# Attention of tile 0 moved ahead of preparation 1, weight splits and raw buffers reordered, a first slot of its own

## The chip, the cores and the metric

The kernel runs on one core of one Trainium2 chip. The metric is the time of one execution on the device in microseconds. All arithmetic is float32; large products are done as three float32r products of high and low parts.

## The reference

Three stages follow one another. The first is a recurrence over 768 tokens for 4 x 8 heads of 48 channels; the second and third are dense layers over the 3072 tokens.

```python
scale = np.minimum(mag, 0.999) / (mag + 1e-06)      # mag = sqrt(a_re^2 + a_im^2)
for t in range(S):
    new_re = ar * S_re - ai * S_im                  # a times the state, complex
    new_im = ar * S_im + ai * S_re
    S_re, S_im = new_re + kv, new_im                # kv = outer(k_t, v_t)
    y[:, :, t] = q_t @ S_re
h = x @ w_in                                        # 384 -> 2048
x = (np.maximum(h, 0) + np.log1p(np.exp(-np.abs(h)))) @ w_out   # -> 384
out = (((x @ w1) * (x @ w2)) @ w3) @ w_out2         # 384 -> 1024 -> 384
```

## The kernel before

The 3072 tokens are cut into eight tiles of 384 tokens. For each tile there are three kinds of work. A *preparation* makes the running products of a (log and root on ScalarE, some 46 us of elementwise work on VectorE), from which q times p and k divided by p are made, stored and loaded back in another layout (stq, stk). The *attention* of a tile has six parts i (three chunks by two groups of heads): `scores` and transposes and `outputs` on TensorE, `mask_scores` and `new_state` on VectorE, `k_by_tokens` and `y_out` on ScalarE, then `store_y` by DMA into x1raw. The *dense layers* of a tile take eight steps j: `up(n, j)` projects x1 by w_in, `softplus` (three passes, ScalarE), `add_relu` (VectorE, L1192), `g_high` (ScalarE, L762), `g_low` (VectorE, L1199) and `down(n, j)` multiplies by w_out.

Engines run their instructions in the order in which they are written, and that order is written by hand. A slot n holds the dense layers of tile n, the attention of tile n + 1 (parts 0 to 5 at steps 0 to 5), the preparation of tile n + 2 and the head of that of tile n + 3. On TensorE a step is `up(n, j+1)`, `scores(n+1, j)`, `down(n, j)`, `outputs(n+1, j)`. The last output product of a slot, `down(n, 7)`, is done in the next slot.

Ahead of slot 0 stands a prologue: TensorE makes w34 = w3 times w_out2 (L1326), and the pieces 0 to 7 of w_in (0 to 3) and w_out (4 to 7) are loaded into three raw buffers and split: `raw_high` on ScalarE (L664), then `raw_low` on VectorE (L1108), after which the buffer is free again. The list RAW says which buffer a piece uses. `load_piece` waits for the raw_low of the buffer's former piece. The raw buffers lie over sp, x1h, x1l and x1raw. VectorE's prologue goes through preparation 0 with raw_low 0 to 3 between its steps, then the head of preparation 1 with raw_low 4 to 6, and only then `mask_scores(0, 0)`; the rest of preparation 1 lies between the parts of the attention of tile 0, its end behind x1_low(0), and preparation 2 is begun before slot 0.

The names of steps on VectorE are: m2 (L950), newton (L957, L960), scale, a (L975), run 1 to 7 and carry 1 to 32 (L941 to L945), by (L1016, L1018), p (L1025, L1026), q (L1035), p2 (L1039), inverse (L1045, L1047), keys (L1052), keys end (L1057). Those on ScalarE are prep_squares (L675), prep_log (L680), prep_root (L684), prep_root_square (L691), prep_psquares (L699) and prep_inverse (L709, L712).

## Time and profile before

| | us |
|---|---|
| median of 3 runs | 989.77 (987.28 to 989.94) |
| the profiled execution, its time | 985.9 |
| the profiled execution, its span | 984.1 |
| TensorE busy | 898.6 (91%) |
| VectorE busy | 608.6 (62%) |
| ScalarE busy | 426.4 (43%) |

The page cuts the span into 40 slices of 24.6 us; each digit is the busy share in tenths, PEclk is TensorE's granted clock in tenths of the full one, where the digit 9 means 90% or more.

```profile
PE   0973739999999999999999999999999999999998
DVE  5978978989898998898999832355221212121211
ACT  4143263585574674664764654587112020202011
PEclk9995668999999999999999999999999999999999
```

TensorE is nearly always busy from slice 7 on. In the slices before it isn't, and its clock is at times half the full one. VectorE is busy in the first 20 slices and lightly used in the last part, which is the third layer. PE is TensorE, PEld its weight loads, DVE VectorE, ACT ScalarE, POOL GpSimd, and SPq the queue from which the DMAs are issued.

### The profile page before, as it was taken

Reading aid. Unit: us, or ns where it says so; the run is one execution under the profiler, and the core shown is the slowest. Engines: PE = TensorE matmul, PEld = TensorE weight load, DVE = VectorE, ACT = ScalarE, POOL = GpSimd, SP = SyncE. Lnnn points to the kernel's source line nnn. Section 1 sums busy time; section 2 is a strip of 40 time slices with the busy share of each in tenths; the row PEclk is TensorE's granted clock in tenths of the full one; section 3 lists DMA queues with packets and bytes.
Section 4 is the critical chain, followed back from the end, with each engine's and each line's share of the span. In section 5 each row is a group of like instructions: output and inputs, shape, how many; then the busy total and the mean of one; then the engine's idle time right before and its main releaser. Section 6 shows DMA issues by size and latency. Waiting matters only on the chain.

```text
span 984.1 us, 14229 instructions
## 1 busy us (share of the span) xinstructions
PE 898.6 (91%) x5298; PEld 800.5 (81%) x5298; DVE 608.6 (62%) x982; ACT 426.4 (43%) x612; POOL 70.0 (7%) x56
## 2 busy tenths in 40 slices
PE   0973739999999999999999999999999999999998
PEld 0543639989989989989889999998888888888887
DVE  5978978989898998898999832355221212121211
ACT  4143263585574674664764654587112020202011
POOL 0000000000000000000000000000222222222221
PEclk9995668999999999999999999999999999999999
DMA  9766065273372381570570550421101010101000
GB/s 336 243 192 192 21 195 130 69 195 99 109 182 74 116 215 36 149 201 13 158 196 12 143 113 13 146 90 47 35 1 65 1 65 1 64 0 64 0 32 33
DMA packets 97878, 99.50 MB, mean 101 GB/s; under 512 B 6928, under 2 KB 88848, under 8 KB 97808
## 3 DMA queue, kind: packets, MB, share of 16 engines
q1 hardware_dynamic: 97808, 98.59, 34.5%
q8 instruction: 41, 0.67, 0.3%
q14 instruction: 29, 0.24, 0.1%
HBM read 63.96 MB, written 29.88 MB: 95 GB/s over the span
## 4 chain that ended last, share of the span: by engine, by line
PE 63%; DVE 21%; ACT 5%; DVEq 5%; issue 3%; DMA 1%; ACTq 1%; SPq 0%
PE ps L1313 8%; PE ps_p L1313 8%; PE ps L1315 8%; PE ps L1314 7%; PE ps_p L1315 7%; PE ps_p L1314 7%; PE ps_ay L1349 3%; DVE sp L1192 2%; DVE an L1018 2%; PE ps_ay L1313 2%; PE ps_ay L1314 2%; PE ps_ay L1315 2%; PE ps_k L1313 2%; PE ps_k L1314 2%; PE ps_k L1315 2%
## 5 line engine op out<-in xcount | busy, mean ns | idle before, releaser
L1313 PE MATMUL ps<-g_h,wo_h 128*128 128x384 f32 x384 | 133.3, 347 | 2.1 <-DVE g_l L1199 2.1
L646 POOL TENSOR_TENSOR abl<-ab,abh 128x512 fp32r<-128x512 f32 x48 | 69.0, 1438 | 907.3 <-DVE abh L1296 907.3
L1315 PE MATMUL ps<-g_h,wo_l 128*128 128x384 f32 x384 | 129.4, 337 | 0.0
L1314 PE MATMUL ps<-g_l,wo_h 128*128 128x384 f32 x384 | 129.2, 336 | 0.0
L1313 PE MATMUL ps_p<-x1h,win_h 128*128 128x384 f32 x336 | 116.9, 348 | 6.2 <-DVE sp L1192 6.2
L1315 PE MATMUL ps_p<-x1h,win_l 128*128 128x384 f32 x336 | 112.6, 335 | 0.0
L1314 PE MATMUL ps_p<-x1l,win_h 128*128 128x384 f32 x336 | 112.5, 335 | 0.0
L1349 PE MATMUL ps_ay<-stq,stk 96*128 96x128 f32 x384 | 55.1, 289 | 37.6 <-DVE am L1141 14.8
L1287 DVE TENSOR_TENSOR ab<-ps_ay,bc 128x512 f32<-128x512 f32 x24 | 16.6, 692 | 114.6 <-ACT bc L914 114.6
L1349 PEld LDWEIGHTS ps_ay<-stq,stk 96*128 96x128 f32 x384 | 52.1, 202 | 40.0 <-issue 25.8
L762 ACT ACTIVATE g_h<-sp 128x768 fp32r<-128x768 f32 (+1 forms) x71 | 55.4, 780 | 66.6 <-DVE sp L1192 66.2
L749 ACT ACTIVATE sp<-ps_p 128x768 f32<-128x768 f32 (+1 forms) x63 | 46.1, 731 | 86.2 <-PE ps_p L1315 86.2
L1287 DVE TENSOR_TENSOR ab<-ps_p,bc 128x512 f32<-128x512 f32 x24 | 16.6, 692 | 104.4 <-ACT bc L914 104.4
L1192 DVE SCALAR_TENSOR_TENSOR sp<-ps_p,sp 128x768 f32<-128x768 f32 (+1 forms) x63 | 54.7, 868 | 35.0 <-ACT sp L755 31.7
L1313 PEld LDWEIGHTS ps<-g_h,wo_h 128*128 128x128 f32 x384 | 72.7, 189 | 3.8 <-DVE g_l L1199 3.7
L1199 DVE TENSOR_TENSOR g_l<-sp,g_h 128x768 fp32r<-128x768 f32 (+1 forms) x71 | 62.4, 878 | 19.2 <-ACT g_h L762 12.6
L1314 PEld LDWEIGHTS ps<-g_l,wo_h 128*128 128x128 f32 x384 | 72.8, 190 | 0.0
L1315 PEld LDWEIGHTS ps<-g_h,wo_l 128*128 128x128 f32 x384 | 72.6, 189 | 0.0
L1313 PEld LDWEIGHTS ps_p<-x1h,win_h 128*128 128x128 f32 x336 | 63.3, 189 | 9.7 <-DVE sp L1192 9.3
L914 ACT ACTIVATE bc<-ps_k 128x512 f32<-128x512 f32 x24 | 14.4, 598 | 123.6 <-PE ps_k L1315 123.6
L914 ACT ACTIVATE bc<-ps_p 128x512 f32<-128x512 f32 x24 | 14.4, 598 | 119.5 <-PE ps_p L1315 119.5
L1314 PEld LDWEIGHTS ps_p<-x1l,win_h 128*128 128x128 f32 x336 | 63.4, 189 | 0.0
(160 smaller groups left out, 1992.3 us busy)
## 6 DMA issues: line engine op xcount, KB each, us to landing
qk_scr<-tt SPq DMA_DIRECT2D x16, 576.0 KB, 4.8
stq<-qk_scr SPq DMA_DIRECT2D x48, 192.0 KB, 4.6
qk_scr<-pp SPq DMA_DIRECT2D x16, 576.0 KB, 4.2
stk<-qk_scr SPq DMA_DIRECT2D x48, 192.0 KB, 4.5
an<-in_a_re SPq DMA_DIRECT2D x8, 576.0 KB, 4.0
an<-in_a_im SPq DMA_DIRECT2D x8, 576.0 KB, 5.2
qk<-in_q SPq DMA_DIRECT2D x8, 576.0 KB, 7.6
qk<-in_k SPq DMA_DIRECT2D x8, 576.0 KB, 8.7
```

The costliest lines, as they stand in the source:

```text
L646: tensor_tensor(abl[:, m % AR, :], ab[:, m % 2, :], abh[:, m % AR, :].bitcast(F32), ALU.subtract).then_inc(ab_lo, 1)
L749: act(buf, ps_u[j][:, us, 0:T], ACT.Abs)
L762: act(g_h[:, j % GR, us, :], sp[:, j % 2, us, :], ACT.Copy).then_inc(g_hi, us.stop - us.start)
L914: act(bc[:, m % 2, :], ps_ab[m % 2][1], ACT.Copy).then_inc(b_ev, 1)
L1018: ve.tensor_tensor(runs[:, c], runs[:, c], carry_of(1), ALU.mult)
L1192: ve.scalar_tensor_tensor(out=buf, in0=ps_u[j][:, us, 0:T], scalar=0.0, in1=buf, op0=ALU.max, op1=ALU.add)\
L1199: ve.tensor_tensor(g_l[:, j % GR, us, :], sp[:, j % 2, us, :], g_h[:, j % GR, us, :].bitcast(F32), ALU.subtract).then_inc(g_lo, us.stop - ...
L1287: ve.tensor_tensor(ab[:, m % 2, :], ps_ab[m % 2][0], bc[:, m % 2, :], ALU.mult).then_inc(ab_mul, 1)
L1313: mm(o, wh, xh, start=start, stop=False)
L1314: mm(o, wh, xl, start=False, stop=False)
L1315: return mm(o, wl, xh, start=False, stop=stop)
L1349: last = mm(ps_a[:, h4, :], stk[0:D2, h, cs], stq[0:D2, h, cs], start=True, stop=True)
```

## The change

Four things change in order only; every instruction of compute and every transfer is still there.

- The raw buffers are used in turn (0, 1, 2, 0, 1, 2, 0, 1). On SP's queue piece 3 is issued before v, piece 4 after the q store, pieces 5 and 6 after the loads of keys, and the y stores wait for six splits instead of five.
- On VectorE raw_low(1) stands behind p2 of preparation 0, raw_low(2) and (3) behind m2 of preparation 1, (4) and (5) just ahead of the first mask, (6) and (7) in parts 0 and 2 of the attention. The attention of tile 0 starts before the runs of preparation 1 and takes them between its parts; three of the products by the carries come after it, and p, q, p2 and the rest after x1_low(0), with the softplus of step 0 between.
- Preparation 2 is begun inside slot 0 (squares at step 0, root at step 1) instead of before it.
- Slot 0 has code of its own on three engines: the attention of tile 1 lies at steps 2 to 7 instead of 0 to 5, down(0, 7) is done in slot 0, and up(1, 0), with the head of preparation 3, comes behind.

```diff
--- before.py
+++ after.py
@@ -103,7 +103,7 @@
         PIECE = 4 * DM
         raw = [sb(f"raw{i}", [P, PIECE], at=at_sp + 4 * PIECE * i)[0] for i in range(3)]
 
-        RAW = [0, 1, 0, 1, 2, 0, 1, 0]
+        RAW = [0, 1, 2, 0, 1, 2, 0, 1]
         w34s, _ = sb("w34s", [P, NM2, DM], at=at_g)
 
         col_t, _ = sb("col_t", [P, CT], I32, at=at_am)
@@ -457,25 +457,27 @@
 
             load_w3(0)
             load_w3(1)
-            load_piece(2)
+            for i in range(2, 4):
+                load_piece(i)
             for c in range(NCH):
                 load_v(0, c)
-            for i in range(3, 7):
-                load_piece(i)
             wait(prep_p, 2)
             load_a(1)
             store_q(0, first=True)
+            load_piece(4)
             for c in range(NCH):
                 stack_q(0, c)
             store_k(0, first=True)
             for c in range(NCH):
                 stack_k(0, c)
+            for i in range(5, 7):
+                load_piece(i)
             load_qk(1)
             wait(w34_ev, NM2)
             eng.dma_start(w34_scr.rearrange("c p n -> p c n"), w34s[:, :, :]).then_inc(w34_wr, 16)
             load_piece(7)
 
-            wait(raw_lo, 5)
+            wait(raw_lo, 6)
             for i in range(NG):
                 store_y(0, i)
             wait(prep_p, 4)
@@ -765,9 +767,8 @@
             raw_high(0)
             prep_log(0)
             prep_rsqrt(0, first=True)
-            raw_high(1)
-            raw_high(2)
-            raw_high(3)
+            for i in range(1, 4):
+                raw_high(i)
             prep_psquares(0)
             prep_inverse(0)
             prep_squares(1)
@@ -775,25 +776,23 @@
             prep_rsqrt(1)
             for mi in range(NM2):
                 w34_rows(mi)
-            for i in range(4, 7):
+            for i in range(4, 6):
                 raw_high(i)
             k_by_tokens(0, 0)
             for i in range(NG):
                 if i + 1 < NG:
                     k_by_tokens(0, i + 1)
                 y_out(0, i, first=True)
-                if i == 1:
-                    raw_high(7)
-            prep_psquares(1)
+                if i in (0, 2):
+                    raw_high(6 + i // 2)
+
             eng.wait_ge(raw_lo, 8)
             for part in range(2):
                 y_loaded(0, part)
                 x1_high(0, part, first=True)
+            prep_psquares(1)
             prep_inverse(1)
-            prep_squares(2)
             softplus(0, 0, False)
-            prep_log(2)
-            prep_rsqrt(2)
             eng.wait_ge(w34_wr, 16)
             g_high(0, 0, False)
 
@@ -868,7 +867,43 @@
                 if not nxt and not weights:
                     x2_out(n)
 
-            slot(0, True, True, True, prev=False)
+            def first_slot():
+
+                for j in range(NP1 - 1):
+                    if j >= 3:
+                        y_out(1, j - 3)
+
+                    def between():
+                        if j == 6:
+                            prep_psquare(2, 0)
+                        if j >= 2:
+                            k_by_tokens(1, j - 2)
+
+                    softplus(0, j + 1, False, between)
+                    if j == 1:
+                        prep_log(2)
+                        prep_root(2)
+                    if j == 6:
+                        prep_psquare(2, 1)
+                    g_high(0, j + 1, False)
+                    if j == 0:
+                        prep_squares(2)
+                    if j == 1:
+                        prep_root_square(2)
+                y_out(1, 4)
+                prep_inverse(2)
+                y_loaded(1, 0)
+                x1_high(1, 0)
+                y_out(1, 5)
+                prep_squares(3)
+                y_loaded(1, 1)
+                x1_high(1, 1)
+                prep_log(3)
+                prep_rsqrt(3)
+                softplus(1, 0, False)
+                g_high(1, 0, False)
+
+            first_slot()
             for n in range(1, NT - 3):
                 slot(n, True, True, True)
             slot(NT - 3, True, True, False)
@@ -1151,33 +1186,32 @@
             tokens_mask()
             prep(0, True, ["m2"])
             raw_low(0)
-            prep(0, True, ["newton", "scale start", "scale"] + steps("a", 0, 1) + steps("run", 1, 2))
+            prep(0, True, ["newton", "scale start", "scale"] + steps("a", 0, 1) + steps("run", 1, 2, 3, 4, 5, 6, 7) +
+                 ["ends"] + steps("carry", 1, 2, 4, 8, 16, 32) + by +
+                 ["p", ("q", 0), ("q", 1), "p2"], first=True)
             raw_low(1)
-            prep(0, True, steps("run", 3, 4, 5, 6, 7))
-            raw_low(2)
-            prep(0, True, ["ends"] + steps("carry", 1, 2, 4))
-            raw_low(3)
-            prep(0, True, steps("carry", 8, 16, 32) + by + ["p", ("q", 0), ("q", 1), "p2", "inverse", "keys", "keys end"], first=True)
-            prep(1, False, ["m2", "newton", "scale start", "scale"] + steps("a", 0, 1))
-            for i in range(4, 7):
-                prep(1, False, steps("run", i - 3))
+            prep(0, True, ["inverse", "keys", "keys end"])
+            prep(1, False, ["m2"])
+            for i in range(2, 4):
                 raw_low(i)
-            prep(1, False, steps("run", 4))
+            prep(1, False, ["newton", "scale start", "scale"] + steps("a", 0, 1))
+            for i in range(4, 6):
+                raw_low(i)
             mask_scores(0, 0)
-            between = [steps("run", 5), steps("run", 6), steps("run", 7), ["ends"] + steps("carry", 1),
-                       steps("carry", 2, 4), steps("carry", 8, 16), steps("carry", 32) + by[:1], by[1:3], by[3:], [], ["p"], []]
+            between = [steps("run", 1), steps("run", 2), steps("run", 3), steps("run", 4), steps("run", 5), steps("run", 6),
+                       steps("run", 7) + ["ends"], steps("carry", 1), steps("carry", 2, 4), steps("carry", 8),
+                       steps("carry", 16, 32), by[:1]]
             for i in range(NG):
                 if i + 1 < NG:
                     mask_scores(0, i + 1)
                 prep(1, False, between[2 * i])
                 new_state(0, i, ps_z0)
                 prep(1, False, between[2 * i + 1])
-                if i == 2:
-                    raw_low(7)
-            prep(1, False, steps("q", 0, 1))
+                if i in (0, 2):
+                    raw_low(6 + i // 2)
+            prep(1, False, by[1:])
             x1_low(0)
-            prep(1, False, ["p2", "inverse", "keys", "keys end"])
-            prep(2, True, ["m2"])
+            prep(1, False, ["p", ("q", 0), "p2", ("q", 1), "inverse"])
 
             def low_x2_first(times):
                 eng.wait_ge(x2f_hi, times)
@@ -1200,8 +1234,9 @@
                                      ALU.subtract).then_inc(g_lo, us.stop - us.start)
 
             add_relu(0, 0, False)
-            prep(2, True, ["newton", "scale start", "scale"] + steps("a", 0))
+            prep(1, False, ["keys"])
             g_low(0, 0, False)
+            prep(1, False, ["keys end"])
 
             def slot(n, att, has_prep, nxt_prep, even, nxt=True, weights=False):
 
@@ -1249,7 +1284,32 @@
                     elif weights:
                         w34_low()
 
-            slot(0, True, True, True, True)
+            def first_slot():
+                for j in range(NP1 - 1):
+                    if j >= 3:
+                        new_state(1, j - 3)
+                    if j >= 2:
+                        prep(2, True, first_before_mask[j - 2])
+                        mask_scores(1, j - 2)
+                        prep(2, True, after_mask[j - 2])
+                    add_relu(0, j + 1, False)
+                    if j >= 2:
+                        prep(2, True, after_sum[j - 2])
+                    g_low(0, j + 1, False)
+                    if j == 0:
+                        prep(2, True, ["m2"])
+                    if j == 1:
+                        prep(2, True, ["newton", "scale start", "scale"])
+                mask_scores(1, 5)
+                prep(2, True, ["inverse", "keys", "keys end"])
+                x1_low(1)
+                prep(3, False, ["m2", "newton", "scale start"])
+                add_relu(1, 0, False)
+                prep(3, False, ["scale"] + steps("a", 0))
+                g_low(1, 0, False)
+
+            first_before_mask = {**before_mask, 0: steps("a", 0, 1)}
+            first_slot()
             for n in range(1, NT - 3):
                 slot(n, True, True, True, n % 2 == 0)
             slot(NT - 3, True, True, False, False)
@@ -1451,9 +1511,19 @@
                     if j == flag_after:
                         all_ok()
 
+
             up(0, 0)
-            slot(0, True, True, prev=False)
-            for n in range(1, NT - 3):
+            for j in range(NP1):
+                if j < NP1 - 1:
+                    up(0, j + 1)
+                if j >= 2:
+                    scores(1, j - 2)
+                down(0, j, False)
+                if j >= 2:
+                    outputs(1, j - 2, False)
+            up(1, 0)
+            slot(1, True, False, prev=False)
+            for n in range(2, NT - 3):
                 slot(n, True, n % 2 == 0)
             slot(NT - 3, True, False)
             slot(NT - 2, True, True)
```

## Rows read from the trace of the kernel before

**Rows 1.** Busy time by stretch: stretch, length, then each engine's busy us, TensorE clock, DMA.

```profile
0.00:91.70 91.70, 46.23 (x140) 27.62 (x140) 71.27 (x115) 31.17 (x36) 0.92 (x8) 0.89 0.80 258
91.70:122.90 31.20, 24.74 (x188) 21.50 (x188) 25.85 (x58) 6.41 (x15) 0.00 (x0) 0.66 0.06 17
122.90:139.30 16.40, 9.30 (x36) 9.01 (x36) 13.14 (x11) 10.64 (x16) 0.00 (x0) 0.67 0.49 161
139.30:222.00 82.70, 71.43 (x486) 67.74 (x487) 72.46 (x114) 47.47 (x64) 0.00 (x0) 0.92 0.58 146
222.00:292.00 70.00, 67.86 (x481) 64.00 (x480) 63.25 (x104) 43.10 (x62) 0.00 (x0) 1.00 0.45 124
```

**Rows 2.** Timeline of TensorE: start, us, instruction, idle before it and its releaser.

```profile
77.39 2.05 PE L1349 MATMUL ps_ay<-stq,stk 96*128 96x128 f32 x8 [10.09 <-DMA stk<-qk_scr]
...
92.51 2.08 PE L1349 MATMUL ps_ay<-stq,stk 96*128 96x128 f32 x8 [12.44 <-DVE am L1141]
...
127.48 0.66 PE L1313 MATMUL ps_ay<-x1h,win_h 128*128 128x384 f32 x1 [4.97 <-DVE x1l L1113]
...
148.21 2.04 PE L1349 MATMUL ps_ay<-stq,stk 96*128 96x128 f32 x8 [11.42 <-DMA vt<-in_v]
```

**Rows 3.** VectorE's waits, 20 to 222 us: us in total, times, longest.

```profile
DVE tr L957 <- ACT tt L691: 6.4, 2, 3.8
DVE tr L1045 <- ACT te L712: 5.1, 2, 2.6
DVE am L1141 <- PE ps_k L1352: 3.7, 2, 2.8
DVE sp L1192 <- ACT sp L755: 1.2, 3, 0.5
DVE state L1149 <- PE ps_p L1381: 1.0, 1, 1.0
```

**Rows 4.** Timeline of VectorE, 41 to 123 us.

```profile
41.23 1.76 DVE L1108 TENSOR_TENSOR win_l<-raw,win_h 128x1536 fp32r<-128x1536 f32 x1
...
60.84 1.36 DVE L1045 TENSOR_TENSOR tr<-te 128x1152 f32<-128x1152 f32 x1 [2.56 <-ACT te L712]
...
72.75 1.36 DVE L957 SCALAR_TENSOR_TENSOR tr<-te,tt 128x1152 f32<-128x1152 f32 x1 [3.76 <-ACT tt L691]
...
91.76 0.69 DVE L1141 TENSOR_TENSOR am<-ps_ay,mask 128x512 f32<-128x512 f32 x1
95.26 0.69 DVE L1141 TENSOR_TENSOR am<-ps_ay,mask 128x512 f32<-128x512 f32 x1 [2.81 <-PE ps_k L1352]
...
122.55 0.35 DVE L1149 TENSOR_TENSOR state<-state,ps_p 96x192 f32<-96x192 f32 x1 [0.97 <-PE ps_p L1381]
```

**Rows 5.** Timeline of SP's queue: loads and stores of keys.

```profile
73.28 2.90 SPq L416 DMA_DIRECT2D stk<-qk_scr  x6
...
137.96 0.89 SPq L401 DMA_DIRECT2D qk_scr<-pp  x2
```

**Rows 6.** DMA issues up to 200 us: issues, KB each, median us to landing.

```profile
raw<-in_w_out SPq DMA_DIRECT2D x4, 768.0 KB, 4.5
```

**Rows 7.** Timeline of ScalarE: first and last pass of a softplus.

```profile
136.25 0.79 ACT L749 ACTIVATE sp<-ps_ay 128x768 f32<-128x768 f32 x1
...
138.02 0.84 ACT L755 ACTIVATE sp<-sp 128x768 f32<-128x768 f32 x1
```

**Rows 8.** Stretches of one us in which TensorE's granted clock changed.

```profile
140.00:141.00 1.00, 0.00 (x0) 0.00 (x0) 0.32 (x1) 0.93 (x2) 0.00 (x0) 0.72 1.04 373
106.00:107.00 1.00, 0.00 (x0) 0.00 (x0) 0.92 (x4) 0.03 (x1) 0.00 (x0) 0.66 0.16 41
```

**Rows 9.** Timeline of VectorE at the end of slot 0.

```profile
213.96 0.96 DVE L1192 SCALAR_TENSOR_TENSOR sp<-ps_p,sp 128x768 f32<-128x768 f32 x1
...
215.98 0.96 DVE L1199 TENSOR_TENSOR g_l<-sp,g_h 128x768 fp32r<-128x768 f32 x1 [0.40 <-ACT g_h L762]
...
221.07 0.96 DVE L1199 TENSOR_TENSOR g_l<-sp,g_h 128x768 fp32r<-128x768 f32 x1
```

## Prediction

> **What bounds the kernel now.** I read first the busy time by stretch, then who waits on TensorE, then who waits on VectorE. In the table of stretches [rows 1] TensorE is busy 67.9 of 70 us from 222 us on: the slots after slot 0 are bound by TensorE, and the change leaves them as they are. So the question is only when slot 1 is reached. The mark that I use is the start of the first output product of slot 1, at 222.5 us, just after VectorE's g_low(1,0), which starts at 221.07 us [rows 9]; both kernels have the same work done at this mark, but for one group.
>
> Before the mark TensorE is idle in three large pieces [rows 2]: 12.4 us until the first mask (its scores were done at 80.1 us), 5.0 us until the first x1l, and 11.4 us until the keys and v of tile 1 have landed. A reader who stops there expects that the change, which goes at the first and the third, brings some 20 us. The VectorE column says otherwise. VectorE is busy 182.7 of the first 222 us, the sum of the first four rows of [rows 1], and the change neither adds nor takes away one VectorE instruction. The mark moves only as far as VectorE's gaps shrink. Before 20 us they are the same in both. From 20 to 222 us its waits come to 20.3 us: 17.4 us in the five rows shown and 2.9 us in eight smaller ones [rows 3]. The rest is small gaps between dependent instructions, which stay. The mask at 91.76 us has no wait on it [rows 4]: it is late because preparation work of tile 1 stands ahead of it on VectorE. Moving it forward gives TensorE an earlier start and VectorE nothing, since the bypassed work must still be done.
>
> **Up to the first mask.** The weight splits (raw_low) of pieces 1 to 3 leave the chain of preparation 0. Each takes 1.76 us, the next instruction begins 1.67 us after its start [rows 4], so the chain ends 3 x 1.67 = 5.0 us earlier. One goes into the wait for the inverse, 2.56 us, of which 0.9 is left. Two go into the wait for the root of tile 1, 3.76 us, of which 0.4 is left [rows 4]. The keys of tile 0 are ready at 62.7, their load is issued at 73.3 - 5.0 = 68.3 us [rows 5], and TensorE has its scores at 72.4 instead of 77.39. VectorE has the factors of tile 1 at 80.7 - 5.0 = 75.7 us and then wants pieces 4 and 5. Piece 5 and piece 6 have now moved in SP's queue behind the six key loads (2.9 us of issuing [rows 5]); piece 5 goes out at 71.4. With the 4.5 us of such a load [rows 6] it lands at 75.9; the key loads ahead of it were still moving until 7.2 us after their first issue, so I take 77.6, and 79.6 as upper end. Then 1.5 us on ScalarE and the split: VectorE waits 1.6 us (0 to 3.6), and the mask comes at 80.7 us, 11 us earlier.
>
> **The attention of tile 0.** It took 31 us, 91.76 to 122.9 [rows 4], with VectorE busy 25.9 of 31.2 us [rows 1]. Of preparation 1, four runs move in and three products and p move out, and one more split moves in: 28.5 us of work instead of 27.3, by the sum of the steps. The 2.81 us until the second scores [rows 4] stay. The split of piece 6 waits 0.4 us for ScalarE, where it stands behind y_out(0); that delays the key copies of part 2 too, beside VectorE's work. The last state update comes at 111.1. Piece 7 and the w34 store are issued earlier and land by about 90 us, before y_out(2) needs a finished y store at 93.8; if they don't, this chain slips by the difference (0 to 2 us). The four products by the carries, 5.2 us, now stand between the last state and x1_low(0), so the first projection starts at 118.0, 9.5 us before the 127.48 of [rows 2]. ScalarE's squares move behind x1_high and cost nothing there.
>
> **To the end of preparation 1.** p, q and p2 follow x1_low. The second q fills half of the inverse's wait of 2.56 us, 1.3 is left. The rest runs on: add_relu(0,0) at 128.6, keys, g_low(0,0) at 130.9, keys end from 131.9 to 134.4. In the kernel before, VectorE stood at the same place at 137.9 (store issued at 137.96 [rows 5]), though with the squared modulus of tile 2 nearly ready. Of the 9.5 us only some 4 are left: the work that was bypassed has been done here.
>
> **Slot 0.** Preparation 2 now starts inside the slot, and its chain is paid in waits:
> - g_low(0,1): between add_relu and g_low lies a ScalarE pass, 2.0 us from start to start [rows 9], and nothing stands between them: 1.2 us. The squares of tile 2 come only then: 1.3 us.
> - add_relu(0,2): up(0,2) starts at 135.4 and ends 3.2 later, the three passes and the hand-over take 2.7 (136.25 to 138.86 [rows 7]), VectorE is free at 140.1: 1.5 us.
> - g_low(0,2) waits for log and root of tile 2, which stand ahead of g_high on ScalarE: 2.6 us, and 0.1 for the last square.
> - steps 2 to 7: VectorE runs behind TensorE with its steps full, and the waits that it had for projection results go. At the end, g_low(0,7) and the inverse cost 1.1 us.
> - after x1_low(1), the squared modulus of tile 3 goes to ScalarE and comes back with nothing to fill the wait, as the one of tile 1 did at 72.75 [rows 4]: 3.8 us.
>
> The key loads of tile 1 are ready 10.3 us after keys end, as before (137.96 to 148.21, [rows 2, 5]), at 144.7; TensorE asks for them at 145.8, so the 11.4 us go, but only from TensorE. On SP the y stores, the next a and the q stores keep their order behind events that are earlier now. Preparation 3's part in the slot is the same work as before.
>
> **The sum.** VectorE's waits after 20 us: 0.9 + 0.4 + 1.6 + 2.8 + 0.4 + 1.3 up to 134.4 us, then 1.2 + 1.3 + 1.5 + 2.6 + 0.1 + 1.1 + 3.8 = 19.0 us, against 20.3. That is 1.3 us won with TensorE at full clock. TensorE itself arrives at the mark with the last output product of slot 0 already done (3.3 us), but waits there for g_low.
>
> **What TensorE's gaps cost.** The granted clock was 0.72 in the microsecond from 140 us, 3.6 us after TensorE's last product at 136.8, so it fell from the higher (2.4 GHz) to the lower level (1.2 GHz) within this gap; it also fell near 106 us, between short products with two gaps of 1.1 and 1.7 us [rows 8]. The change opens new gaps: 4.9 us before down(0,0) at 132.0, 4.2 us before outputs(1,0), 5.7 before up(1,0). Down(0,0), 18 products in 3.3 us, would at half the clock end 2.0 us late if the clock comes back after 5 us of work and 3.3 late if not; up(0,2), on whose result VectorE waits, follows it: I take +2.0 us on the mark. Outputs(1,0) and up(0,4) at the lower level would cost another 0 to 2.1. The gap before up(1,0) is covered by the 3.8 us wait, +0.2 at most. I take +2.0 for the first, which is longer than the 3.6 us, and nothing for the second, which is on the border and has VectorE's queue as cover.
> The Trainium skill (TensorE: Matmul & The Clock Gate, "Part 1: The HAM clock gate") says that the throttled state is the default and activity releases it; taken strictly it would charge every one of these gaps, and the mark would come -1.3 + 2.0 + 2.1 + 0.2 = 3.0 us late rather than 0.7. The trace agrees as far as 140 us goes; no row shows a gap of 4 to 5 us inside a slot.
>
> So the mark moves by -1.3 + 2.0 = +0.7 us, and the slots behind it, bound by TensorE, keep that. The profiled execution has a span of 984.1 and a time of 985.9 us; it gives 986.6. It lay 3.9 us below the median of 989.77, a spread as large as the effects here. On the median: 990.5 us.
>
> **Rivals.**
> 1. No measurable change, the forecast: within 0.3% (3.0 us), which is about what a measurement of this kernel can tell from none. 0.45.
> 2. TensorE sets the pace in slot 0. For it speak its 71.4 us busy of 82.7 [rows 1]; against it VectorE's total. If the bypassed work found cover everywhere, the start of the first projection 9.5 us earlier and the 11.4 us load wait would both count: -15 to -18 us, 973. Chance 0.04. In part: the piece lands at once (-1.6), the clock stays up (-2.0), g_low(0,1) and the log find half of their waits filled (-2.5): -3 to -6 us, 985. Chance 0.18.
> 3. Slower: the clock falls in both gaps at the head of slot 0 and VectorE, which never catches up there, passes it all on: 0.7 + 2.1, and one to three us more if slot 1 also starts at the lower level, since it is bound by TensorE: 992.6 to 996. It decides from the point where the idle time before down(0,0) and outputs(1,0) is over 3.6 us. Chance 0.26.
> 4. The change doesn't do what it says: piece 5 lands late behind key loads and stores, the mask comes at 84 us and not 80.7, and every microsecond passes on: +3 to +5 us, 993 to 995. Chance 0.07.
>
> Faster than 0.3%: 0.04 + 0.18 = 0.22. Same: 0.45. Slower: 0.26 + 0.07 = 0.33. The range takes the waits with bounds: below -1.6, -2.0 and -2.5 around the forecast, above +2 (piece), +2.1 (second gap), +2 (slot 1 or y stores): 984.5 to 996.
>
> **What would show it.** Mask of tile 0 at 80 to 82 us, VectorE's state update at 111, first projection at 118, keys end of tile 1 at 134, scores of tile 1 at 146 without a DMA wait; a VectorE wait of about 3.8 us for the root of tile 3; g_low(1,0) at 221 to 222 us. VectorE's busy time up to the mark should be 183 us in both. I am wrong if g_low(1,0) comes at 216 or earlier, or if VectorE shows waits in steps 3 to 6 of slot 0; then TensorE or ScalarE sets the pace there.

## The result, and the profile after

The changed kernel takes 996.83 us (996.72 to 997.98, 4 runs), the kernel before, beside it, 989.85 (987.28 to 989.94, 4 runs). The ratio is 1.0085, with an interval of 1.0069 to 1.01: slower by 7 us, and just outside the predicted range. The profiled execution of after has a span of 994.9 and a time of 996.72 us. The two profiled executions are further apart than the medians, 10.8 us by their spans, because that of before lies 3.9 us below its median. Everything that is read from the two profiles below adds up to the 10.8 us and not to the 7.0; why that execution of before was the shorter one, no trace shows.

TensorE's two rows in the page of after, which answer to those of before (slices of 24.9 us):

```profile
PE   0977578968999999999999999999999999999998
...
PEclk9995688978999999999999999999999999999999
```

In slices 3 to 6 TensorE reads 7757, where before it read 7373: the first mask comes earlier and the wait for the keys of tile 1 is gone. In slices 7, 9 and 10 it reads 8, 6 and 8, where before there stood 9s. The table of stretches gives VectorE up to its g_low(1,0), the mark of the prediction, which starts at 221.07 us before [rows 9] and at 229.66 after. Columns as in [rows 1]; the row of before:

```profile
0.00:222.00 222.00, 151.69 (x850) 125.87 (x851) 182.72 (x296) 95.70 (x128) 0.92 (x8) 0.85 0.59 175
```

And the row of after:

```profile
0.00:230.60 230.60, 161.27 (x856) 135.26 (x856) 183.02 (x296) 97.76 (x130) 0.93 (x8) 0.84 0.59 173
```

The same 296 instructions, 182.7 and 183.0 us of them, in a stretch that is 8.6 us longer. So it is VectorE's waits again, from 20 to 230 us of after (us in total, times, longest), against the 20.3 us of [rows 3]:

```profile
DVE am L1176 <- PE ps_k L1412: 4.7, 3, 2.8
DVE sp L1226 <- ACT sp L757: 4.5, 3, 3.8
DVE tr L992 <- ACT tt L693: 4.0, 2, 3.8
DVE g_l L1233 <- ACT g_h L764: 3.4, 2, 2.3
DVE wo_l L1143 <- ACT wo_h L666: 3.3, 2, 2.4
DVE tr L1080 <- ACT te L714: 2.7, 3, 1.1
DVE x1l L1148 <- ACT x1h L721: 1.9, 1, 1.9
DVE state L1184 <- PE ps_p L1441: 1.7, 2, 1.3
```

With four smaller ones of 2.2 us they come to 28.4 us, 8.1 more than before. The wait for the root (tr L992, before L957) has lost 2.4 us and that for the inverse (L1080) as much; these are the waits that the moved work fills. The other six rows are new or have grown. The timeline of VectorE of after shows the first places, which answer to [rows 4], and then two in slot 0, add_relu(0,2) and mask(1,1) (start, us, instruction, idle before it and its releaser):

```profile
80.18 1.76 DVE L1143 TENSOR_TENSOR wo_l<-raw,wo_h 128x1536 fp32r<-128x1536 f32 x1 [2.38 <-ACT wo_h L666]
81.86 0.68 DVE L1176 TENSOR_TENSOR am<-ps_ay,mask 128x512 f32<-128x512 f32 x1
...
114.03 0.35 DVE L1184 TENSOR_TENSOR state<-state,ps_p 96x192 f32<-96x192 f32 x1 [0.39 <-PE ps_p L1441]
...
146.83 0.96 DVE L1226 SCALAR_TENSOR_TENSOR sp<-ps_p,sp 128x768 f32<-128x768 f32 x1 [3.77 <-ACT sp L757]
...
169.49 0.69 DVE L1176 TENSOR_TENSOR am<-ps_ay,mask 128x512 f32<-128x512 f32 x1 [1.65 <-PE ps_k L1412]
```

The mask of tile 0 starts at 81.86 instead of 91.76 us, and the last state update at 114.03 instead of 122.55. The timeline of TensorE of after, at its gaps:

```profile
121.05 0.66 PE L1373 MATMUL ps_ay<-x1h,win_h 128*128 128x384 f32 x1 [7.06 <-DVE x1l L1148]
...
135.14 0.69 PE L1373 MATMUL ps<-g_h,wo_h 128*128 128x384 f32 x1 [5.06 <-DVE g_l L1233]
...
160.01 0.43 PE L1432 MATMUL ps_ay<-stq,state 96*48 96x128 f32 x4 [4.39 <-DVE am L1176]
...
205.46 0.69 PE L1373 MATMUL ps<-g_h,wo_h 128*128 128x384 f32 x1 [2.86 <-DVE g_l L1233]
...
217.11 0.69 PE L1373 MATMUL ps_ay<-x1h,win_h 128*128 128x384 f32 x1 [5.85 <-DVE x1l L1148]
...
230.68 0.69 PE L1373 MATMUL ps<-g_h,wo_h 128*128 128x384 f32 x1 [2.03 <-DVE g_l L1233]
```

Of the large gaps of [rows 2] the one of 12.4 us is 6.9 us long now, the one of 5.0 has grown to 7.1, and the one of 11.4 is gone: the scores of tile 1 start at 151.07 us with no wait for a DMA. Behind them stand new gaps of 5.1, 4.4, 2.9, 5.9 and 2.0 us, each released by VectorE. At all five the clock fell from the higher to the lower level: in the gap itself at four of them, and at the one of 4.4 us at about 160.7 us, when the products had run again for 0.7 us. Stretches of after, with the columns as above; the clock is the last number but two:

```profile
160.00:161.00 1.00, 0.99 (x16) 0.90 (x16) 0.93 (x4) 0.00 (x0) 0.00 (x0) 0.86 0.05 16
161.00:167.00 6.00, 6.00 (x26) 5.75 (x23) 5.49 (x14) 1.12 (x2) 0.00 (x0) 0.50 0.05 14
230.00:236.00 6.00, 5.32 (x17) 5.33 (x18) 5.63 (x11) 2.48 (x4) 0.00 (x0) 0.51 0.54 194
```

Slot 1 of before, from add_relu(1,0) to the x1_high at its end:

```profile
218.70:279.70 61.00, 60.11 (x441) 56.88 (x440) 55.12 (x95) 36.27 (x53) 0.00 (x0) 1.00 0.42 115
```

And the stretch between the same two instructions in after:

```profile
225.90:290.30 64.40, 60.20 (x425) 56.78 (x425) 56.48 (x96) 36.33 (x54) 0.00 (x0) 0.95 0.36 99
```

TensorE's clock was at the lower level from 161 to 167 us, behind the second gap, and again from 230 to 236 us, and this stretch takes 64.4 us at a mean of 0.95 instead of 61.0 at 1.00. The two don't hold quite the same work: in before down(0,7), an output product, falls into it, and in after one VectorE instruction of 1.36 us more. Counted from the mark, g_low(1,0), they do: 58.6 us before (221.07 to 279.7) and 60.6 after (229.66 to 290.27), 2.0 us more. That x1_high comes 10.6 us later than in before, at 290.27, and every later one stays 10.6 us later (361.07 against 350.49, 432.19 against 421.58): behind it TensorE is the bound, and it keeps what it is given.

The last of the new waits is at the end of slot 0. ScalarE's timeline of after there:

```profile
215.94 0.52 ACT L721 ACTIVATE x1h<-x1raw 128x384 fp32r<-128x384 f32 x1 [1.96 <-DMA x1raw<-ys]
```

SP's queue ahead of it (start, us of issuing, the transfers):

```profile
207.82 1.04 SPq L409 DMA_DIRECT2D stq<-qk_scr  x2
...
211.72 1.31 SPq L423 DMA_DIRECT2D x1raw<-ys  x2
```

The store of the last part of y of tile 1 is issued at 211.72 us, behind six q and v loads that begin at 207.82, and has landed 4.2 us later; x1_high waits for it, and x1_low (the 1.9 us of x1l above) for x1_high.

### The profile page after: what moved, and what is told of

Same layout as the page of the kernel before. It is cut to its first block, busy times and chain, and to the rows that moved or that the text cites. A ratio compares the mean times of both kernels' runs of the same rounds, so it can differ in the third digit from the quotient of the medians.

```text
span 994.9 us, 14229 instructions
## 1 busy us (share of the span) xinstructions
PE 910.1 (91%) x5298; PEld 811.9 (82%) x5298; DVE 609.0 (61%) x982; ACT 427.5 (43%) x612; POOL 70.0 (7%) x56
## 4 chain that ended last, share of the span: by engine, by line
PE 60%; DVE 21%; ACT 6%; DVEq 6%; issue 3%; DMA 2%; ACTq 1%; SPq 0%
PE ps L1373 7%; PE ps L1375 7%; PE ps L1374 7%; PE ps_p L1373 7%; PE ps_p L1375 7%; PE ps_p L1374 7%; PE ps_ay L1409 3%; DVE sp L1226 2%; PE ps_ay L1375 2%; PE ps_ay L1374 2%; PE ps_ay L1373 2%; DVE an L1053 2%; PE ps_k L1375 2%; PE ps_k L1374 2%; PE ps_k L1373 2%
## 5 line engine op out<-in xcount | busy, mean ns | idle before, releaser
L1373 PE MATMUL ps<-g_h,wo_h 128*128 128x384 f32 x384 | 135.3, 352 | 11.6 <-DVE g_l L1233 11.6
```

What stands on the lines that cost most here:

```text
L1373: mm(o, wh, xh, start=start, stop=False)
```

## The experiments

All ratios are to the kernel before in the same comparison; its medians there were 988.56 for the first four kernels, 988.0 for the next four and 987.74 us for the last two. Against 988.56 the changed kernel lies 8.3 us higher, against its own comparison 7.0: a difference of 1 us between kernels of different comparisons tells nothing.

### The new prologue alone

Everything up to the softplus of step 0 as in after, slot 0 as in before, preparation 2 begun ahead of it as in before.

```diff
-            prep(1, False, ["p", ("q", 0), "p2", ("q", 1), "inverse"])
+            prep(1, False, ["p", ("q", 0), "p2", ("q", 1), "inverse", "keys", "keys end"])
+            prep(2, True, ["m2"])
...
-            first_slot()
+            slot(0, True, True, True, True)
```

> The new prologue alone (buffers in turn, weight splits moved, attention of tile 0 ahead of preparation 1), with slot 0 as in the kernel before. Theory A (VectorE carries the bypassed work, so the earlier mask is worth only the VectorE waits it fills; the loss lies in the new slot 0): keys end of tile 1 some 1 to 2 us before the 137.9 us of the kernel before, mark at the end of slot 0 1 to 3 us earlier, 987 to 989. Rival B (the prologue itself costs, since its pieces land late and the parts of the attention run at the lower clock): 991 or more. Rival C (the first projection 6 us earlier counts): 983 or less.

Measured: 985.36 us (980.66 to 988.98) against 988.56, ratio 0.9967 [0.995, 0.9983]. The wait for piece 5 is larger than in after, and TensorE still waits for the loads of tile 1 (VectorE's timeline of this kernel first):

```profile
82.53 1.76 DVE L1110 TENSOR_TENSOR wo_l<-raw,wo_h 128x1536 fp32r<-128x1536 f32 x1 [4.73 <-ACT wo_h L666]
```

TensorE:

```profile
148.76 1.62 PE L1351 MATMUL ps_ay<-stq,stk 96*128 96x128 f32 x6 [16.38 <-DMA vt<-in_v]
```

What follows: the mask comes some 8 us earlier, at 84.2, TensorE's gap behind the first scores shrinks from 12.4 to 6.8 us, and the kernel wins 3.2 us by the medians: 985.36 us lies between the 987 to 989 of theory A and the 983 or less of rival C, nearer to the first. By the two profiles it wins 0.5 us only (spans 984.1 and 983.6, g_low(1,0) 0.4 us earlier), since the profiled execution of before lies that far below its median. The store of the keys of tile 1 is issued at the same 138 us as before. The bypassed work comes back, as the prediction had it.

### The new slot 0 alone

The prologue as in before, `first_slot` of all three engines as in after, with keys and keys end around g_low(0,0).

```diff
-            prep(1, False, ["p2", "inverse", "keys", "keys end"])
-            prep(2, True, ["m2"])
+            prep(1, False, ["p2", "inverse"])
...
-            slot(0, True, True, True, True)
+            first_slot()
```

> The new slot 0 alone (attention of tile 1 at steps 2 to 7, preparation 2 begun inside the slot), with the prologue of the kernel before. Theory A: VectorE starts the slot at the same time as before but has the waits of a preparation's head uncovered and TensorE falls to the lower clock in its gaps: 997 to 1000, that is 7 to 10 us slower than the kernel before. Rival B (the loss is in the prologue): within 3 us of the kernel before.

Measured: 1002.52 us (1000.99 to 1002.99), ratio 1.0144 [1.0127, 1.0161]. Its waits on VectorE in slot 0 are nearly those of after; the four largest there:

```profile
151.88 0.96 DVE L1224 SCALAR_TENSOR_TENSOR sp<-ps_p,sp 128x768 f32<-128x768 f32 x1 [2.85 <-ACT sp L755]
155.16 0.96 DVE L1231 TENSOR_TENSOR g_l<-sp,g_h 128x768 fp32r<-128x768 f32 x1 [2.32 <-ACT g_h L762]
...
221.52 0.56 DVE L1146 TENSOR_TENSOR x1l<-x1raw,x1h 128x384 fp32r<-128x384 f32 x1 [2.04 <-ACT x1h L719]
...
227.11 1.36 DVE L990 SCALAR_TENSOR_TENSOR tr<-te,tt 128x1152 f32<-128x1152 f32 x1 [3.76 <-ACT tt L691]
```

What follows: the loss is in the new slot, 14 us by itself, more than the 7 to 10 us that were expected. The two parts don't add up to the whole (-3.2 and +14.0 give +10.8, and both together +7.0 to +8.3); what the traces show of the difference stands under Open below.

### TensorE kept at work in its gaps

After, with 88 products more whose results are thrown away: 26 ahead of down(0,0), 22 ahead of outputs(1,0), 14 ahead of down(0,7), 26 ahead of up(1,0).

```diff
+                if j == 0:
+                    eng.wait_ge(x2_ev, 1)
+                    fill(ps_2[:, 0, 0:T], 26)
...
+                if j == 2:
+                    fill(ps_ay[:, 1, 0:T], 22)
...
+            eng.wait_ge(a_masked, NG * 2)
+            fill(ps_ay[:, 0, 0:T], 26)
             up(1, 0)
```

> The changed kernel with 88 products of 384 columns more on TensorE, whose results are thrown away, in four gaps of slot 0: before down(0,0), before outputs(1,0), before down(0,7) and before up(1,0). They take 4.6, 3.9, 2.5 and 4.6 us at the higher clock, so they end before what TensorE waits for. Theory A (2.0 us of the loss from the clock at down(0,0), 2.0 at outputs(1,0) and up(0,4), up to 2 at outputs(1,5), 2.2 in slot 1): 989 to 992, and the granted clock stays at the higher level in slot 0 from 137 us on. Rival D (the clock has no part; VectorE's waits come from ScalarE's passes): 997 or more.

Measured: 993.52 us (993.03 to 996.01), ratio 1.0055 [1.0041, 1.007], 3.3 us under after. The stretch from 137 to 204 us, in after:

```profile
137.00:204.00 67.00, 60.47 (x406) 57.57 (x404) 53.43 (x97) 32.39 (x43) 0.00 (x0) 0.92 0.43 106
```

This kernel:

```profile
137.00:204.00 67.00, 64.29 (x452) 61.14 (x451) 56.49 (x100) 35.21 (x47) 0.00 (x0) 1.00 0.48 122
```

Two waits of VectorE in it:

```profile
145.52 0.96 DVE L1226 SCALAR_TENSOR_TENSOR sp<-ps_p,sp 128x768 f32<-128x768 f32 x1 [1.67 <-ACT sp L757]
...
214.64 0.56 DVE L1148 TENSOR_TENSOR x1l<-x1raw,x1h 128x384 fp32r<-128x384 f32 x1 [3.31 <-ACT x1h L721]
```

What follows: the clock stays at 1.00, the wait at add_relu(0,2) is 1.67 and not 3.77 us, the one at mask(1,1) is gone, and g_low(0,7) starts at 201.16 instead of 204.44 us though slot 0 began 0.8 us later: 4.1 us in slot 0 are the clock. Then the wait for the last y store grows from 1.91 to 3.31 us, and the clock still falls ahead of slot 1. So the theory of the clock holds for slot 0, a part of the gain is handed to the next wait, and the 989 to 992 us of the expectation were missed.

### Pieces 5 and 6 ahead of the key loads

After, with one pair of lines of SP's queue in the other order.

```diff
             store_k(0, first=True)
+            for i in range(5, 7):
+                load_piece(i)
             for c in range(NCH):
                 stack_k(0, c)
-            for i in range(5, 7):
-                load_piece(i)
```

> The changed kernel with pieces 5 and 6 issued ahead of the key loads of tile 0 instead of behind them. Theory A: VectorE's wait of 2.4 us for the high part of piece 5 and that of 0.9 us for piece 6 shrink to under 1 us together, the key loads come some 4 us later but still 2 us before the mask; 994 to 995. If the key loads were needed as they come, the first scores are the new wait and the time stays at 997.

Measured: 993.71 us (992.85 to 994.86), ratio 1.0055 [1.0042, 1.0069], 3.1 us under after. No wait for piece 5 is left; the mask now waits for its scores, whose keys load later (its timeline of VectorE):

```profile
80.90 0.69 DVE L1176 TENSOR_TENSOR am<-ps_ay,mask 128x512 f32<-128x512 f32 x1 [1.49 <-PE ps_k L1412]
```

What follows: rival 4 named a real cost, and it grows on its way. By the two profiles (spans 991.1 and 994.9) the mask comes 1.0 us earlier, the wait of a state update falls from 1.30 to 0.35 and the one at add_relu(0,2) from 3.77 to 2.84 us, both on TensorE's side, and g_low(1,0) starts 3.2 us earlier, at 226.45. The second expectation was right in that the first scores are the new wait, and wrong in the time. At add_relu(0,2) the 0.9 us come from where the clock stands: it is back at the higher level 3.1 us after down(0,0) began here, and 5.1 us after it in after. Nor is the state update's 0.95 us due to the pieces alone: its wait is 0.35 us in the last kernel below, whose pieces load as in after, and 1.30 us in the last but one, whose pieces load early. Both are read from the traces and were not tested by themselves.

### The y store ahead of the q and v loads

After, with the store of part 5 of tile 1 issued before these loads.

```diff
+                    if first:
+                        store_y(n + 1, NG - 1)
                     for c in range(2):
                         stack_q(n + 2, c)
                         load_v(n + 2, c)
-                if att:
+                if att and not first:
                     store_y(n + 1, NG - 1)
```

> The changed kernel with the y store of the last part of tile 1 issued ahead of the loads of q and v of tile 2 in slot 0. In the trace of the changed kernel VectorE waited 1.9 us for the second part of x1 high, whose y store landed 4.2 us after its issue, behind those loads. Theory A (the store's place in SP's queue makes it late): this wait goes to under 0.5 us and the mark comes 1.5 to 2 us earlier, 994.5 to 995.5. Rival (the late outputs(1,5) alone make it late, or the transfers in flight slow it wherever it stands): the wait stays over 1.2 us, 996 to 997.

Measured: 998.33 us (997.33 to 1000.66) against 988.0, ratio 1.0107 [1.0092, 1.0122]. SP's queue in this kernel, at the loads:

```profile
215.36 1.10 SPq L409 DMA_DIRECT2D stq<-qk_scr  x2
```

TensorE in the same kernel:

```profile
231.62 1.62 PE L1411 MATMUL ps_ay<-stq,stk 96*128 96x128 f32 x6 [5.80 <-DMA stk<-qk_scr]
```

What follows: the wait fell as expected and the time was missed. The wait for the y store falls from 1.91 to 0.44 us, but the q loads, formerly issued at 207.82, go out at 215.36 (the queue stands still until part 5 is done), and TensorE waits 5.8 us for the keys of tile 2: from g_low(1,0) on slot 1 takes 62.5 us instead of 60.6. This profile also has 4.76 us of wait for piece 5 where after has 2.38, with the same queue up to there, so 2.4 us of its longer time have nothing to do with the edit. The 1.5 us of the y store were real and not to be had in this way.

### Products thrown away in slot 1 too

The kernel with the 88 products, with the y store moved as above, 34 products ahead of up(1,0) instead of 26, 7 ahead of scores(2,0) and 10 ahead of down(1,0).

```diff
-            fill(ps_ay[:, 0, 0:T], 26)
+            fill(ps_ay[:, 0, 0:T], 34)
...
+                        eng.wait_ge(s_new, states(n + 1, 0))
+                        fill(ps_k[:, 0:T], 7)
...
+                    if warm and j == 0:
+                        fill(ps_ay[:, 1, 0:T], 10)
```

> As e3_fill with the y store of e7_ystore, and with thrown-away products also at the head of slot 1: 34 instead of 26 ahead of up(1,0), 7 ahead of scores(2,0), 10 ahead of down(1,0). Theory A (slot 1 lost 2 to 3 us because its first products ran at the lower clock): the clock stays up through the head of slot 1, the time from add_relu(1,0) to x1 high of tile 2 goes from 64.4 us back to some 61 to 62, and the whole comes to 988 to 990. Rival (slot 1 is longer for another reason): 992 or more.

Measured: 994.12 us (992.39 to 994.94) against 988.0, ratio 1.0062 [1.005, 1.0074]. The stretch up to the end of slot 1:

```profile
137.00:284.00 147.00, 140.47 (x991) 133.39 (x991) 125.93 (x205) 81.65 (x114) 0.00 (x0) 1.00 0.49 126
```

TensorE's timeline in the same kernel:

```profile
223.60 1.13 PE L1411 MATMUL ps_ay<-stq,stk 96*128 96x128 f32 x8 [2.96 <-DMA stk<-qk_scr]
```

What follows: the clock is 1.00 throughout, and slot 1, add_relu(1,0) to x1_high, takes 62.8 us instead of 64.4 with a wait of 2.96 us for keys in it. From g_low(1,0) on it is 59.0 us, against 60.6 in after and 58.6 in before. So the clock costs at least 1.6 us there. The whole doesn't get better than the kernel with 88 products, since the keys' wait takes the place: the 988 to 990 us of the expectation were missed.

### The new prologue alone, with the pieces early

The first experiment and the fourth together (the diffs are shown there).

> The new prologue alone, with pieces 5 and 6 issued ahead of the key loads. Theory A (VectorE sets the time of the prologue, and the wait for piece 5 was part of it): 2 to 3 us less than the new prologue alone, 982 to 984. If slot 0 is held by something else, the keys of tile 1 for one, the time stays at 985 to 986.

Measured: 981.94 us (979.38 to 983.07) against 988.0, ratio 0.9933 [0.9919, 0.9948]: faster than before and than after. VectorE's timeline of it:

```profile
81.04 0.69 DVE L1143 TENSOR_TENSOR am<-ps_ay,mask 128x512 f32<-128x512 f32 x1 [1.56 <-PE ps_k L1354]
```

TensorE in the same kernel:

```profile
144.62 2.04 PE L1351 MATMUL ps_ay<-stq,stk 96*128 96x128 f32 x8 [16.98 <-DMA vt<-in_v]
```

What follows: the 4.73 us of the first experiment have become 1.56, 3.2 us of VectorE's waits are gone, and the kernel is 3.4 us faster than that one (3.3 by the spans, 980.3 and 983.6). TensorE's gap of 17 us ahead of scores(1,0) is larger than the 11.4 of before, and the kernel is faster all the same. In this pair idle time of TensorE counts for nothing, and VectorE's counts one to one. The 4.73 us of the first experiment are at the upper end of what the profiles show for this wait, so how much of the 3.2 us is the price of the order and how much this spread is open.

### The first output product ahead of the scores

The last kernel, with down(0,0) ahead of scores(1,0), g_low(0,0) ahead of keys end and the head of preparation 2 behind.

```diff
+                    if not prev and att and j == 0:
+                        down(n, j, not att)
                     if att and j < NG:
                         scores(n + 1, j)
```

> As e9_prologue_pieces, and in slot 0 TensorE makes down(0,0) ahead of scores(1,0), in the time in which it waits for the keys of tile 1; VectorE makes g_low(0,0) ahead of keys end of tile 1 and the whole head of preparation 2 behind it. Theory A (slot 0 of the kernel before is bound by TensorE, with VectorE close behind): TensorE has 3.3 to 5 us less to do once the keys are there, VectorE gets 2 us more of waits at the head; -1 to -3 us against e9_prologue_pieces. Rival (VectorE is bound there too): 0 to +2 us.

Measured: 984.82 us (983.75 to 986.68) against 988.0, ratio 0.9971 [0.996, 0.9982], 2.9 us over the kernel that it is made from. Its timeline of VectorE:

```profile
140.96 1.36 DVE L959 SCALAR_TENSOR_TENSOR tr<-te,tt 128x1152 f32<-128x1152 f32 x1 [3.76 <-ACT tt L693]
```

TensorE in the same kernel:

```profile
146.50 1.83 PE L1352 MATMUL ps_ay<-stq,stk 96*128 96x128 f32 x7 [8.07 <-DMA stk<-qk_scr]
```

What follows: the long gap is cut in two, 5.9 and 8.1 us, the clock falls all the same, and the root of tile 2 costs VectorE 3.76 us where it was 2.63. Filling TensorE's gap won nothing; the loss is even larger than the 0 to 2 us of the rival.

### The q and v loads of tile 1 ahead of the key store

The last kernel but one, with SP's queue changed.

```diff
             store_q(1)
-            store_k(1)
             wait(yz_mm, NG)
             for c in range(NCH):
                 stack_q(1, c)
-                stack_k(1, c)
                 load_v(1, c)
+            store_k(1)
+            for c in range(NCH):
+                stack_k(1, c)
```

> As e9_prologue_pieces, with the loads of q and v of tile 1 issued ahead of the store and the loads of its keys, so that only the keys are behind keys end. TensorE's wait for v in slot 0 was 17 us. Theory A (what TensorE wins there VectorE doesn't give back: its mask of tile 1 has no wait and g_low(0,0) comes at the same time): the scores come 1 to 2 us earlier, the time is within 1 us of e9_prologue_pieces, 981 to 983. Rival (slot 0 of the kernel before is held by the keys and v): -2 us or more, 980 or less.

Measured: 985.77 us (983.88 to 988.56) against 987.74, ratio 0.9978 [0.9966, 0.9989], 3.8 us over the kernel that it is made from. SP's queue, key store and key loads:

```profile
135.49 0.91 SPq L401 DMA_DIRECT2D qk_scr<-pp  x2
143.71 2.89 SPq L416 DMA_DIRECT2D stk<-qk_scr  x6
```

TensorE in the same kernel:

```profile
147.86 2.05 PE L1352 MATMUL ps_ay<-stq,stk 96*128 96x128 f32 x8 [19.68 <-DMA stk<-qk_scr]
```

What follows: both expectations missed. The key store, now behind six loads, is followed by the first key load after 8.2 us (135.49 to 143.71) instead of 5.5 (134.07 to 139.53), so the keys come later than they did behind it, and VectorE waits 2.41 us for the scores. By the spans (982.8 and 980.3) it is 2.5 us.

### The head of preparation 2 ahead of slot 0

After, with squares, log, root, newton and scale of preparation 2 before slot 0, the attention of tile 1 still at steps 2 to 7.

```diff
+            prep(2, True, ["m2", "newton", "scale start", "scale"] + steps("a", 0))
...
-                    if j == 0:
-                        prep(2, True, ["m2"])
-                    if j == 1:
-                        prep(2, True, ["newton", "scale start", "scale"])
...
-            first_before_mask = {**before_mask, 0: steps("a", 0, 1)}
+            first_before_mask = before_mask
```

> The changed kernel with the head of preparation 2 (squares, log, root, and VectorE's steps up to the first a) ahead of slot 0 again, and the attention of tile 1 still at steps 2 to 7. If the uncovered waits of that head inside the slot are what slot 0 lost, 989 to 992. If the two steps without attention at its start and the mask, inverse and key work crowded at its end are what it lost (the waits at the head only change their place): 995 to 999.

Measured: 1000.97 us (999.92 to 1002.07) against 987.74, ratio 1.0128 [1.011, 1.0145]. VectorE's timeline of it:

```profile
142.04 1.36 DVE L988 SCALAR_TENSOR_TENSOR tr<-te,tt 128x1152 f32<-128x1152 f32 x1 [3.76 <-ACT tt L693]
...
158.25 0.96 DVE L1222 SCALAR_TENSOR_TENSOR sp<-ps_p,sp 128x768 f32<-128x768 f32 x1 [6.59 <-ACT sp L757]
```

What follows: the waits of steps 0 and 1 don't go away with the work that stood in them, they change place and grow (6.59 us at one add_relu). It took 1001 us, more than either expected range. On ScalarE the squares, log and root stand behind g_high(0,0) here and ahead of softplus(0,1), where the kernel before has the squares ahead of softplus(0,0). So the run doesn't restore the order of before; it shows that in this order steps 0 and 1, without attention, have nothing that hides the root and a softplus, and not that no order would.

## Why the prediction was wrong

The frame held: VectorE's waits carry the mark, and the account closes in them: 20.3 us before, 28.4 after, 8.1 us more for a mark 8.6 us later, with 0.3 us of busy time. The prediction had 19.0 us of waits and 2.0 for the clock, which shows as a wait too: 21.0. The missing 7.4 us, and the 2 us behind the mark, step by step:

| step of the prediction | foreseen | measured, us |
|---|---|---|
| wait for piece 5, mask of tile 0 | 1.6, at 80.7 | 2.38, at 81.86 |
| split of piece 6 | 0.4 | 0.94 |
| last state update | no wait, 111.1 | 1.7 in two waits, 114.03 |
| first projection, keys end | 118.0, 134.4 | 121.05, 137.5 |
| lower clock at down(0,0) | +2.0 | add_relu(0,2) waits 3.77 for 1.5 |
| g_low(0,1), squares, g_low(0,2) | 1.2, 1.3, 2.6 | 1.06, 1.27, 2.32 |
| gap ahead of outputs(1,0) | 4.2, cost 0 | 4.39, cost 1.65 + 0.42 |
| gap ahead of down(0,7) | not listed | 2.86 |
| g_low(0,7) and inverse | 1.1 | 0.16 + 0.84 |
| last y store | 0 | 1.91 |
| root of tile 3 | 3.8 | 3.76 |
| slot 1 from the mark on | 0 | +2.0 (10.6 - 8.6) |

**Right.** That an earlier mask wins only what it saves in VectorE's waits: the first and the seventh kernel show it, the first with 3.2 us (0.5 by the profiles) for 8 us of mask, the seventh with 3.4 us more for 3.2 us fewer of waits. That the new slot pays for preparation 2 in waits: g_low(0,1), squares, g_low(0,2), the end of the slot and the root of tile 3 came within 0.3 us of their size, and add_relu(0,2), 1.5 foreseen, is 1.67 us once the clock is kept up. That TensorE's first gap in the slot brings the clock down and costs some 2 us: the wait is 3.77 us, and 1.67 with the clock up. The size has some luck in it: half the speed for 5 us of work, the prediction's own premise, costs 2.5 us and not 2.0.

**Wrong, first: the second gap.** The step "I take ... nothing for the second, which is on the border and has VectorE's queue as cover" failed. The clock fell there too, and VectorE had no cover: it waited 1.65 us at mask(1,1) and 0.42 at the next add_relu. The bound of 2.1 us that stood beside it was the right price, and the row on which it rested, a fall of the clock 3.6 us after the last product, spoke for it, as the foreseen gap of 4.2 us was longer. But these 3.6 us are one reading and no limit: in after the clock fell 2.5 to 5.1 us after the last product at the four gaps of slot 0, one of them, 2.86 us ahead of down(0,7), not listed in the prediction at all. The kernel with 88 products shows the sum of both, 4.1 us against the 2 foreseen. It is also the sign that the prediction had set itself: VectorE waits in steps 3 to 6 of slot 0.

**Wrong, second: slot 1.** "The slots behind it, bound by TensorE, keep that" took no cost behind the mark, and rival 3 had "one to three us more". Measured are 2.0 us, from a clock that fell ahead of up(1,0) and again after 229 us; keeping it up gave back 1.6 us, in spite of a new wait. The prediction looked only at the gap that a wait of VectorE covers and not at what the lower clock does to the products behind it.

**Wrong, third: the last y store.** No step priced it; only the upper bound had "+2 (slot 1 or y stores)", and both came. "On SP the y stores ... keep their order behind events that are earlier now" was true of the order and not of the time: parts 4 and 5 of the attention now lie at steps 6 and 7, so the last y store follows the loads of q and v by 1 us and is needed at once. It costs 1.9 us, of which 1.5 go when the store is issued ahead of the loads; that experiment exchanged them for a wait for the keys. The low clock at down(0,7) has a part in it that no run separates: the last y_out starts 6.9 us after g_low(0,7) in after and 5.5 us after it in the kernel with 88 products.

**Wrong in size: the prologue.** Its waits were 10.7 us instead of 7.4. Rival 4 named the place (piece 5 behind the key loads): 0.8 us more than foreseen in the profile of after, and the other profiles with this prologue have 2.6 to 4.8 us for it, so the bound of 3.6 was too low. The 1.7 us at the state updates were not foreseen at all; their size changes from kernel to kernel with the moment at which the clock comes back.

Added up: -1.3 + 2.0 foreseen, + 3.3 (prologue) + 2.0 (second gap) + 1.9 (y store) + 0.2 in small ones = 8.1 us of waits, then 2.0 us in slot 1. That is the account of the two profiles, where the forecast was 986.6 us and 996.72 came. By the medians, 990.5 foreseen and 996.83 measured, only 6.3 us are missing: the other 3.8 are the spread of the kernel before, whose profiled execution lies so far below its median. They are no effect of the change, and no trace puts them on single steps. The mechanism is rival 3's, which was given 0.26 and 992.6 to 996 us; with rival 4's it passes the upper end. The two are not exclusive, and the prediction counted them as if they were. The range's own upper terms (+2, +2.1 and +2 on 990.5) give 996.6 and not 996; the measured time is outside either.

**Open.** The two halves give 2.5 to 3.8 us more apart than together (3.8 by the spans). The traces show where it lies and not all of why: for piece 5 the first kernel waits 4.73 us and after 2.38, with the same order of the queue; the second kernel waits 1.39 and 0.84 us at two masks of tile 0 (after: 0.23 at one) and 1.91 at add_relu(0,0) (after: 0.17), and 0.9 us less at add_relu(0,2). How much of the loss of the new slot beyond clock and y store is due to steps 0 and 1 is open too: the last kernel moves their waits and doesn't price them.

## What to carry to other kernels

Sum the waits of the engine that sets the time up to the point where the bound changes, not the idle time of the one downstream: moving work ahead of other work of the same engine only turns waits around. Price every new gap of TensorE, with the products behind it, at the lower clock, and add the mishaps of a forecast that can happen together. Compare the profiled execution with its own median before a forecast is put on it. For a transfer that changes place in a queue, look at what then stands right ahead of it and at who is next to wait.

## What the runs showed of the hardware

- The granted clock fell 3.3 us after TensorE's last product in a gap of 5.1 us, 4.1 us after it in one of 5.9 and 2.5 us after it in one of 2.9; behind a gap of 4.4 us it fell 5.1 us after the last product of before the gap, when the next products had run for 0.7 us; and at 229.0 us it fell 0.4 us into a gap of 2.03 us that followed one of 1.25. In the kernel with products thrown away in slot 1 too, a gap of 2.96 us left it at 1.00, and the clock was 1.00 from 137 to 284 us. So the length of a gap alone didn't tell here whether the clock fell. The Trainium skill (TensorE: Matmul & The Clock Gate, "Part 1: The HAM clock gate") has the throttled state as the default that activity releases, and the trace agrees in that the clock fell at all of these places but the 2.96 us.
- Two y stores of 48 KB landed 3.6 us after their issue behind q and v loads, and 2.0 us after it where the loads stood behind them. A key store behind six such loads was followed by its first load after 8.2 us instead of 5.5. A small transfer took longer with larger ones issued just ahead of it.
- The wait for the same piece of weights was 2.4 to 3.1 us in four profiles and 4.7 to 4.8 in two others of kernels with the same order of the queue.
